# First tiles of a fused attention and mixture-of-experts kernel: no table for roots, decay loaded first, three clamps on VectorE, queries scaled ahead of a clamp, and unread turns of the unit matrix on TensorE

## The reference

```python
f = 1.0 / (1.0 + np.exp(-f_logit))                       # attention: B=4, H=8, S=768, D=48
for t in range(S):
    state = f[:, :, t, :, None] * state + np.einsum('bhd,bhe->bhde', k[:, :, t], v[:, :, t])
    y[:, :, t] = np.einsum('bhd,bhde->bhe', q[:, :, t], state)

xn = x / (np.linalg.norm(x, axis=-1, keepdims=True) + 1e-06)          # experts: E=8, rows of 384
en = expert_emb / (np.linalg.norm(expert_emb, axis=-1, keepdims=True) + 1e-06)
logits = xn @ en.T / tau
...
```

## Time and profile before

| what | value |
|---|---|
| median of 3 runs | 761.31 us (760.79 to 761.64) |
| the profiled execution, its own time | 764.95 us |
| its span, first to last instruction | 763.2 us |
| PE busy in the span | 724.4 us (95%) |
| DVE, ACT, POOL busy | 322.9, 281.6, 212.5 us |
| granted TensorE clock, mean of the span | 0.985 |
| attention stage | to about 154 us |

### The profile page before, as it was taken

The page is one execution under the profiler, slowest core; times in us unless marked ns, Lnnn a source line. Parts: engine busy times, 40 slices in busy tenths (PEclk is TensorE's granted clock), DMA queues, the critical chain, the costliest instruction groups (busy, mean ns, idle before and its releaser), DMA issues.

```text
span 763.2 us, 13668 instructions
## 1 busy us (share of the span) xinstructions
PE 724.4 (95%) x4832; PEld 646.6 (85%) x4832; DVE 322.9 (42%) x528; ACT 281.6 (37%) x520; POOL 212.5 (28%) x246
## 2 busy tenths in 40 slices
PE   4999999999479999999999989999999999999995
PEld 3999999856279999999999988898988988889885
DVE  5667777557135564564554651211211212112110
ACT  6666666423034354453453542302213022121220
POOL 7656756317700000000000002305224042141341
PEclk9999999999779999999999999999999999999998
DMA  8677885264824453552553451001000000000001
GB/s 252 183 230 212 267 231 136 75 187 152 283 54 125 124 166 96 152 165 82 159 153 100 132 146 55 1 1 41 1 17 24 0 31 10 4 38 0 21 21 41
DMA packets 78542, 79.51 MB, mean 104 GB/s; under 512 B 20688, under 2 KB 66776, under 8 KB 78512
## 3 DMA queue, kind: packets, MB, share of 16 engines
q1 hardware_dynamic: 75184, 68.88, 30.6%
q0 software_dynamic: 3328, 10.25, 3.7%
HBM read 64.09 MB, written 15.02 MB: 104 GB/s over the span
## 4 chain that ended last, share of the span: by engine, by line
PE 68%; issue 15%; POOL 11%; another core or an unknown queue 3%; ACT 1%; DVE 0%; POOLq 0%; DVEq 0%
PE bank L760 9%; PE bank L762 9%; PE bank L761 9%; POOL p_lo L583 7%; PE b_a L760 6%; PE b_a L761 6%; PE b_a L762 6%; PE b_a L620 4%; PE bank L629 3%; PE bank L660 3%; POOL out L588 3%; PE b_a L730 3%; PE bank L669 3%; PE bank L649 3%
## 5 line engine op out<-in xcount | busy, mean ns | idle before, releaser
L583 POOL TENSOR_TENSOR p_lo<-prod,p_hi 128x512 fp32r<-128x512 f32 x48 | 61.5, 1286 | 441.5 <-ACT p_hi L1003 441.5
L1000 ACT COPY a_sb<-b_a 128x512 f32<-128x512 f32 x48 | 28.3, 589 | 222.9 <-PE bank L762 222.9
L1335 DVE TENSOR_TENSOR prod<-bank,a_sb 128x512 f32<-128x512 f32 x48 | 33.2, 692 | 163.9 <-ACT a_sb L1000 163.9
L760 PE MATMUL b_a<-x_hi,w_hi 128*128 128x432 f32 x192 | 69.7, 363 | 15.3 <-DVE w_lo L1230 15.3
L965 ACT ACTIVATE h_hi<-b_a 128x432 fp32r<-128x432 f32 x64 | 34.1, 532 | 120.4 <-PE b_a L762 120.4
L1299 DVE SCALAR_TENSOR_TENSOR h_lo<-b_a,h_hi 128x432 fp32r<-128x432 f32 x64 | 38.9, 607 | 89.6 <-ACT h_hi L965 89.6
L1230 DVE TENSOR_TENSOR w_lo<-w_raw,w_hi 128x768 fp32r<-128x768 f32 x72 | 67.8, 957 | 6.6
L760 PE MATMUL bank<-h_hi,w_hi 128*128 128x432 f32 x192 | 70.1, 365 | 0.0
L761 PE MATMUL b_a<-x_lo,w_hi 128*128 128x432 f32 x192 | 69.5, 362 | 0.0
L762 PE MATMUL b_a<-x_hi,w_lo 128*128 128x432 f32 x192 | 69.4, 361 | 0.0
L762 PE MATMUL bank<-h_hi,w_lo 128*128 128x432 f32 x192 | 68.7, 358 | 0.0
(11 more groups left out here) (199 smaller groups left out, 1433.2 us busy)
## 6 DMA issues: line engine op xcount, KB each, us to landing
w_raw<-sets SPq DMA_DIRECT2D x80, 192.0 KB
w_raw<-sets SPq DMA_DIRECT2D x40, 384.0 KB
ring_all<-qkvf SPq DMA_DIRECT2D x24, 384.0 KB, 4.1
xs<-x_sorted SPq DMA_DIRECT2D x9, 772.0 KB, 6.0
ring_f<-qkvf SPq DMA_DIRECT2D x24, 192.0 KB, 4.0
ring_all<-qkvf SPq DMA_DIRECT2D x24, 192.0 KB, 3.2
x_recurrence<-x_all SPq DMA_DIRECT2D x24, 192.0 KB, 3.6
w_sb<-w_t SPq DMA_DIRECT2D x8, 512.0 KB, 4.9
```

What stands on the lines that cost most here:

```text
L583: pool.tensor_tensor(p_lo[:, f, :], prod[:, f % 2, :], p_hi[:, f, :].bitcast(F32), ALU.subtract).then_inc(pl_done, 1)
L760: pe.matmul(acc, a_hi, b_hi, start=first, stop=False, skip_group_check=skip)
L1000: act.copy(a_sb[:, f % 2, :], b_a[f % 2][:]).then_inc(as_done, 1)
L1335: dve.tensor_tensor(prod[:, f % 2, :], b_b[f % 2][:], a_sb[:, f % 2, :], ALU.mult).then_inc(pr_done, 1)
```

## The change

- The embedding is loaded fourth, not first. It lands in `x_tile`, with its squares in `rt`. The root is no longer ACT's Sqrt, so that one table load of ACT is gone: ACT takes Ln and Exp of half of it in step -1 (`guess_norm`), and DVE improves the guess in step 0 with one step of Newton's method and divides (`scale_emb`, seven instructions, five of them linked by a semaphore each). PE turns the embedding behind `turn_qk` of tile 1, not of tile 0.
- SP's order is decay of tile 0, queries and keys of tile 0, decay of tile 1, embedding, decay of tile 2. The load of `tau` and the four blocks of zeros stand behind the stages of tiles 4 to 7. The reciprocal of `tau` is taken on DVE behind all steps.
- DVE clamps tiles 0, 1 and 2, the first two right after its first memset. Tile 1's `low_logs` moves into step -2, behind `bound` of tile 0. POOL clamps from tile 3 on, so that `scale_q` of tile 0 is its first instruction behind the constants.
- ACT copies `qT` of tile 0 ahead of `exps` of tile 1.
- PE transposes the unit matrix into `b_x`, which nobody reads: 16 times at the start, 10 times between `cumulate` of tiles 0 and 1, and 8 times ahead of `turn_qk` of tile 0.

```diff
@@ -287,8 +287,6 @@
...
-        sp.dma_start(emb_sb, emb).then_inc(emb_in, 16)
...
@@ -337,10 +335,10 @@
...
         load_f(0, 0)
+        load_qk(0, 0)
         load_f(1, 1)
-        load_qk(0, 0)
+        sp.dma_start(emb_sb, emb).then_inc(emb_in, 16)
         load_f(2, 2)
-        sp.dma_start(tau_sb[:], tau).then_inc(small_in, 16)
         load_qk(1, 1)
         load_v(0, 0)
...
         load_v(RING - 1, RING - 1)
-        sp.wait_ge(pads_done, 3)
-        for i in range(SUB):
-            sp.dma_start(xs_dram[NTOK + i * P:NTOK + (i + 1) * P, :], zero_rows[:]).then_inc(zero_out, 16)
...
@@ -375,6 +370,10 @@
...
         four(1)
+        sp.dma_start(tau_sb[:], tau).then_inc(small_in, 16)
+        sp.wait_ge(pads_done, 3)
+        for i in range(SUB):
+            sp.dma_start(xs_dram[NTOK + i * P:NTOK + (i + 1) * P, :], zero_rows[:]).then_inc(zero_out, 16)
         with sp.Fori(2, NT // RING - 1) as m:
...
@@ -485,7 +484,7 @@
...
-            need(pool, lg_done, i if isinstance(i, int) and i == 2 else i - 1)
+            need(pool, lg_done, i if isinstance(i, int) and i == 3 else i - 1)
...
@@ -510,11 +509,11 @@
...
         def step(s, r):
-            if (i := tile_of(s, 3, 2)) is not None:
+            if (i := tile_of(s, 3, 3)) is not None:
                 before_clamp(i, r + 3)
             if (i := tile_of(s, -2)) is not None:
                 decay(i, r + 2)
-            if (i := tile_of(s, 3, 2)) is not None:
+            if (i := tile_of(s, 3, 3)) is not None:
                 clamp(i, r + 3)
             if (i := tile_of(s, 1)) is not None:
                 scale_q(i, r + 1)
@@ -604,6 +603,11 @@
...
+        def warm(n):
+
+            for _ in range(n):
+                pe.transpose(b_x[:, 0:P], ident[:], ident[:])
+
...
         def turn_emb():
 
-            pe.wait_ge(emb_step, 4)
+            pe.wait_ge(emb_scaled, 1)
...
         def step(s, r):
+            if isinstance(s, int) and s < 0:
+                warm({-3: 16, -2: 0, -1: 10}[s])
             if (i := tile_of(s, 0)) is not None:
                 scores(i, r)
             if (i := tile_of(s, 2)) is not None:
@@ -703,8 +709,9 @@
             if (i := tile_of(s, 1)) is not None:
                 if isinstance(i, int) and i == 0:
                     pe.wait_ge(pads_done, 1)
+                    warm(8)
                 turn_qk(i, r + 1)
-                if isinstance(i, int) and i == 0:
+                if isinstance(i, int) and i == 1:
                     turn_emb()
...
@@ -860,9 +867,6 @@
...
-        act.wait_ge(emb_step, 1)
-        act.activation(emb_n[:, 1:2], emb_n[:, 0:1], ACT.Sqrt).then_inc(emb_step, 1)
...
@@ -892,6 +896,13 @@
...
+        def guess_norm():
+
+            act.wait_ge(emb_step, 1)
+            act.activation(emb_n[:, 1:2], emb_n[:, 0:1], ACT.Ln).then_inc(emb_step, 1)
+            act.wait_ge(emb_step, 2)
+            act.activation(emb_n[:, 2:3], emb_n[:, 1:2], ACT.Exp, scale=0.5).then_inc(emb_step, 1)
...
                 copy_yT(i)
             if (i := tile_of(s, 3, 2)) is not None:
                 logs(i, r + 3)
+            if isinstance(s, int) and s == -1:
+                copy_qT(0, 0)
             if (i := tile_of(s, 2)) is not None:
                 exps(i, r + 2)
-            if (i := tile_of(s, 1)) is not None:
+            if isinstance(s, int) and s == -1:
+                guess_norm()
+            if (i := tile_of(s, 1, 1)) is not None:
                 copy_qT(i, r + 1)
...
@@ -1025,9 +1040,6 @@
...
-        dve.wait_ge(emb_in, 16)
-        dve.tensor_tensor_reduce(out=emb_sq, in0=emb_sb, in1=emb_sb, scale=1.0, scalar=0.0,
-                                 op0=ALU.mult, op1=ALU.add, accum_out=emb_n[:, 0:1]).then_inc(emb_step, 1)
...
@@ -1083,11 +1095,15 @@
...
-            if (i := tile_of(s, 3, 2)) is not None:
+            if (i := tile_of(s, 3, 1)) is not None:
                 low_logs(i, r + 3)
+            if isinstance(s, int) and s == -3:
+                first_clamp(2)
+            if isinstance(s, int) and s == 0:
+                scale_emb()
             if (i := tile_of(s, 1)) is not None:
                 copy_kT(i, r + 1)
-                if isinstance(i, int) and i == 0:
+                if isinstance(i, int) and i == 1:
                     take_emb()
...
         def first_clamp(i):
 
             dve.wait_ge(f_landed[i], 16)
-            dve.tensor_scalar_max(fc[:, i, :], ring_f[:, i, :], FLOOR).then_inc(clamp_done, 1)
+            need(dve, lg_done, i - 1)
+            dve.tensor_scalar_max(fc[:, i % 2, :], ring_f[:, i, :], FLOOR).then_inc(clamp_done, 1)
...
+        def scale_emb():
+
+            dve.wait_ge(emb_step, 3)
+            link(dve.reciprocal(emb_n[:, 3:4], emb_n[:, 2:3]))
+            link(dve.tensor_tensor(emb_n[:, 4:5], emb_n[:, 3:4], emb_n[:, 0:1], ALU.mult))
+            link(dve.tensor_tensor(emb_n[:, 5:6], emb_n[:, 4:5], emb_n[:, 2:3], ALU.add))
+            link(dve.tensor_scalar(emb_n[:, 6:7], emb_n[:, 5:6], 0.5, EPS_NORM, ALU.mult, ALU.add))
+            link(dve.reciprocal(emb_n[:, 7:8], emb_n[:, 6:7]))
+            dve.tensor_scalar(emb_pad[:, :, 0:D], emb_sb.rearrange("p (h d) -> p h d", h=H), emb_n[:, 7:8], None, ALU.mult)
+            dve.tensor_scalar(emb_sq, emb_sb, emb_n[:, 7:8], None, ALU.mult).then_inc(emb_scaled, 1)
+
         dve.memset(b_y[:], 0.0).then_inc(blank_done, 1)
+        first_clamp(0)
+        first_clamp(1)
         dve.memset(yT[:], 0.0).then_inc(blank_done, 1)
         dve.wait_ge(masks_done, 3)
         dve.tensor_copy(upto_r[:], upto[:])
-        first_clamp(0)
-        first_clamp(1)
         dve.tensor_copy(pick[:, :, 0:2 * D].rearrange("p j (g d) -> p j g d", g=2),
                         ident[:].rearrange("p (g d) -> p g d", g=2)[:, :, 0:D].unsqueeze(1).to_broadcast([P, NP, 2, D]))
-        dve.wait_ge(emb_step, 2)
-        link(dve.tensor_scalar_add(emb_n[:, 2:3], emb_n[:, 1:2], EPS_NORM))
-        dve.reciprocal(emb_n[:, 3:4], emb_n[:, 2:3]).then_inc(emb_step, 1)
         low_logs(0, 0)
-        dve.wait_ge(emb_step, 3)
-        dve.wait_ge(blank_done, 2)
-        dve.tensor_scalar(emb_pad[:, :, 0:D], emb_sb.rearrange("p (h d) -> p h d", h=H), emb_n[:, 3:4], None, ALU.mult)
-        dve.tensor_scalar(emb_sq, emb_sb, emb_n[:, 3:4], None, ALU.mult).then_inc(emb_step, 1)
-        low_logs(1, 1)
+        dve.wait_ge(emb_in, 16)
+        dve.tensor_tensor_reduce(out=emb_sq, in0=emb_sb, in1=emb_sb, scale=1.0, scalar=TINY,
+                                 op0=ALU.mult, op1=ALU.add, accum_out=emb_n[:, 0:1]).then_inc(emb_step, 1)
+        dve.wait_ge(pads_done, 2)
+        steps(dve, step)
+
+        dve.wait_ge(const_done, 1)
         dve.wait_ge(small_in, 16)
         link(dve.reciprocal(rtau[:], tau_sb[:]))
-        dve.wait_ge(pads_done, 2)
-        steps(dve, step)
-
-        dve.wait_ge(const_done, 1)
```

More of the change, by code:

```diff
@@ L56 @@
 EPS_SUM = 1e-9
+TINY = 1e-30
 RING = 4
@@ L161, in build @@
     en_t = early("en_t", [P, KD, E])
-    emb_sb = am[0:E, 0].rearrange("p j t -> p (j t)")[:, 0:DM]
-    emb_sq = am[0:E, 1].rearrange("p j t -> p (j t)")[:, 0:DM]
     emb_pad = yT[0:E, :].rearrange("p (h d) -> p h d", h=H)
-    emb_n = early("emb_n", [E, 4])
+    emb_n = early("emb_n", [E, 8])
     tau_sb = early("tau_sb", [P, 1])
@@ L181, in build @@
     zero_rows = early("zero_rows", [P, ROW])
+    emb_sb, emb_sq = x_tile[0:E, :], rt[0:E, 0:DM]
     x_rows = x_all[:, 0:NT * ROW]
@@ L251, in build @@
     masks_done, pads_done = sem("masks_done"), sem("pads_done")
-    const_one, const_done, emb_step, emb_turned, en_done = (sem(n) for n in (
-        "const_one", "const_done", "emb_step", "emb_turned", "en_done"))
+    const_one, const_done, emb_step, emb_scaled, emb_turned, en_done = (sem(n) for n in (
+        "const_one", "const_done", "emb_step", "emb_scaled", "emb_turned", "en_done"))
     clamp_done, ef_done, lg_done, ll_done, cum_done, bound_done, ec_done, exp_done = (sem(n) for n in (
@@ L1111, in _ @@
         dve.tensor_copy(upto_r[:], upto[:])
-        first_clamp(0)
-        first_clamp(1)
         dve.tensor_copy(pick[:, :, 0:2 * D].rearrange("p j (g d) -> p j g d", g=2),
                         ident[:].rearrange("p (g d) -> p g d", g=2)[:, :, 0:D].unsqueeze(1).to_broadcast([P, NP, 2, D]))
-        dve.wait_ge(emb_step, 2)
-        link(dve.tensor_scalar_add(emb_n[:, 2:3], emb_n[:, 1:2], EPS_NORM))
-        dve.reciprocal(emb_n[:, 3:4], emb_n[:, 2:3]).then_inc(emb_step, 1)
         low_logs(0, 0)
-        dve.wait_ge(emb_step, 3)
-        dve.wait_ge(blank_done, 2)
-        dve.tensor_scalar(emb_pad[:, :, 0:D], emb_sb.rearrange("p (h d) -> p h d", h=H), emb_n[:, 3:4], None, ALU.mult)
-        dve.tensor_scalar(emb_sq, emb_sb, emb_n[:, 3:4], None, ALU.mult).then_inc(emb_step, 1)
-        low_logs(1, 1)
-        dve.wait_ge(small_in, 16)
-        link(dve.reciprocal(rtau[:], tau_sb[:]))
+        dve.wait_ge(emb_in, 16)
+        dve.tensor_tensor_reduce(out=emb_sq, in0=emb_sb, in1=emb_sb, scale=1.0, scalar=TINY,
```

(3 more changed lines are left out.)

## The result

The changed kernel takes 766.82 us (median of 4 executions, 766.17 to 768.52), the kernel before 761.35 in the same session (4, 760.79 to 761.64): a ratio of 1.0077, with an interval of 1.0061 to 1.0093. Forecast were 760.1 and a range to 763.9, so the time lies outside it, on the slow side. The profiled execution took 766.59 with a span of 764.8.

The account below looks back on a forecast made before the run. TensorE bounds the kernel, busy 724.4 of 763.2 us. Scores of tile 1 1.4 us earlier plus 0.2 for 1/tau gave -1.2 us: 760.1 against the median 761.31, 8-in-10 range 759.1 to 763.9.

Parts of the forecast that it names:

- step 6: Embedding's new place: TensorE stands 2.65 us ahead of its turn; scores of tile 1 at 20.75, 1.4 us earlier.
- the premise that behind the scores of tile 1 nothing changes: Behind the start of tile 1's scores, engines have the work of before at TensorE's pace: 5.73 us per tile.
- Steps 1 to 3: Program start: third load at 5.8, sums at 7.6, `ec` at 9.3, queries at 9.45 in place of 10.56.
- step 2: VectorE to the first sums: GpSimd's constants, ending at 9.42, just cover the late clamp; loads later than 5.8 cost fully.
- The clock in the pause: Rival: clock rises early, falls in the pause ahead of the embedding's turn; products cost 1.0 more, 761.1; chance 0.10.
- Step 4: The 34 unread turns: first 16 free; the other 18 take 0.11 us each at high clock, 4.4 us at low.
- The rival built on that rule: Clock comes late or not from transposes: +2.8 to +3.8 us, 764.1 to 765.1; chance 0.15.
- Step 5: Tile 0 at high clock: turns 10.85 to 11.7, scores at 12.55 in place of 14.51, 1.95 us won.
- Step 7: The rest: zeros and `tau` moved to the middle are covered by load lead; 1/tau on VectorE adds 0.17 us.

Follow-up runs that it names:

- Experiment 4: Changed kernel with the decay of tile 1 loaded second, ahead of queries and keys of tile 0: ratio 1.0068 against the kernel before.
- experiment 6: Changed kernel with 24 more unread turns in TensorE's pause, right ahead of the embedding's turn: ratio 1.0106 against the kernel before.
- experiments 9: Changed kernel with the 10 and 8 turns taken out and 18 put into the pause ahead of the embedding's turn: ratio 1.0041 against the kernel before.
- 11: The kernel of numbers 10 with only the first 16 turns, without the 10 and the 8: ratio 1.0012 against the kernel before.
- number 7: Changed kernel with the embedding prepared one step earlier and decay of tile 1 loaded second: 758.83 us, ratio 0.9964 against the kernel before.
- experiment 12: Kernel before with the same 34 turns (16, 10, 8) and nothing else of the change: ratio 0.9976 against the kernel before.
- numbers 10: The kernel of number 7 with 1/tau taken on VectorE at the end of an earlier step: ratio 0.9964 against the kernel before.

## Why the prediction was wrong, point by point

**The step that failed is step 6 with what it left out of the clock,** and with it the premise that behind the scores of tile 1 nothing changes. The place and kind of the loss were right (a pause ahead of the embedding's turn, products and the copy of `kT` queued behind it), and so was the early clock. Against 20.75 for the scores of tile 1 the chain has 23.91, 3.16 more, and it splits into three:

- Steps 1 to 3, 0.67 (scores of tile 0 at 13.22, not 12.55). The third load was clamped at 6.29, not 5.8, inside its bounds. From there to the start of `lg_lo` it took 1.36 us, not 1.1, most of the difference in the copy of `pick` (0.46 on the path, counted at 0.27). `ec` ended at 10.0 for 9.3, and GpSimd's constants, the cover I named, were over at 8.75 for 9.42: it waited 1.35 us. Once the cover was gone each late tenth was on the path, as step 2 had said. Experiment 4 shows the price: up to 1.5 us at the sums. The landing itself isn't fixed: with this order of loads the clamp began between 4.97 and 6.29 in seven executions.
- Step 6's sum of operations, 0.9. From the scores of tile 0 to the embedding's turn it took 6.12 us, not 5.2. The mask began 0.5 late, behind VectorE's product for the keys of tile 1; the small operation beside GpSimd's product was 0.75 longer than the 0.15 of its neighbours; the two scalings took 0.75 where I had 1.02.
- The clock in the pause, 1.64. I gave it a chance of 0.10 and a price of 1.0; experiment 6 measured 1.64. The embedding's own turns were 0.60 (0.65 forecast). All three executions with a pause of 3.5 us show the fall; with this pause filled or gone, none has it there.

**Step 4** was right. The 16 turns raised the clock: sums of 0.44 us behind them, in eight of the ten executions with these turns. The Trainium skill ("TensorE: Matmul & The Clock Gate", Part 4: PE-mode transpose) says that the full clock does not engage for transposes; the measurement differs and decides. The rival built on that rule got 0.15 and foresaw a slower kernel, but by another way than the one that happened. Right, too, was that 10 and 8 turns cost little; that without them the clock is low again, or stays low, for tile 0 I had not seen (experiments 9 and 11).

**Step 5** had the turns (0.89), the 0.87 to the scores and the early rise. **Step 7** was right: from the scores of tile 1 to `least_e` it is 132.67 us against 132.50, so 1/tau cost its 0.2 and the zeros in the middle nothing. Wrong was the premise ahead of the steps, that behind tile 1 "the engines have the work of before": the loss at tile 1 is 2.5 us against the repeated kernel before, and the span's is 5.8. Apart from 1/tau it is two falls of the clock, at 157 and at 457. They can be read off as two levels. From the first dense matmul to the end it takes 307.5 to 307.7 us in seven executions, and 309.2 to 309.3 in six (309.2 in the changed kernel: 764.8 - 455.59); experiment 6 stands apart (310.1). Likewise it takes 1.6 to 1.7 us more in five of fourteen to a point 12 us behind `least_e`. This is the view of the windows with the fall and without it, in number 7 and in the repeat of before:

```profile
449.00:452.00 3.00, 3.00 (x9) 2.32 (x8) 0.00 (x0) 0.00 (x0) 0.00 (x0) 0.50 1.05 335
```

```profile
456.00:460.00 4.00, 4.00 (x19) 3.30 (x19) 0.69 (x1) 0.56 (x2) 0.00 (x0) 1.00 0.16 59
```

The sum against the repeat of before: 2.5 at tile 1, 0.2 for 1/tau, 1.5 from `least_e` to the dense groups (with the fall at 157) and 1.6 behind (with that at 457) make 5.8, the difference of the spans. Only the first two are shown to be the change's. The fast kernel of experiment 7 has the fall at 449 as well, the kernel before with turns (experiment 12) has both, and the two executions of the changed kernel differ in it; so whether the change makes these later falls more frequent, or this execution drew both, stays open. In the repeat of the changed kernel the loss at tile 1 was 4.3 and one later fall 1.7. Of the 6.7 us by which the forecast missed, then, step 6 and its neighbours hold 3.2, and most of the rest lies in these later falls, for which the sum had no term.

**The baseline.** I took -1.2 off a profiled execution that held a stand of 17 us on ScalarE, 3.5 us of it on the path. The difference was carried over, so the stand itself did no harm. But that execution also began 0.7 us later than its repeat (22.07 and 21.37 at tile 1), so half of the forecast gain of 1.4 was measured against a late start, and the one trace could not show that the clock's falls are drawn anew, and the earlier trace rows were read behind that stand.

## What to carry to other kernels

Filling work that raises TensorE's clock is worth only what the next pause leaves of it: look for the first place where TensorE waits, and move what it waits for (here seven small operations of VectorE, 4.8 us at tile 1) before adding any filler. When a pause is estimated, price its upper end with the work behind it at the low clock. And take two profiled executions before working with differences of 1 us, since the clock's falls behind equal pauses came in some and not in others, at 1.5 to 1.7 us each.

## What was not expected of the hardware

- Transposes of the unit matrix alone raised the granted clock: after 16 in 3.68 us, sums took 0.44 us, not the 0.66 to 0.69 without them. It was not certain: in one kernel two executions differed by the second sums (0.44 and 0.69), and in numbers 10 and 11 the first sums still took 0.69, where number 7, the same to that point, has 0.44.
- Pauses of 2.3 to 2.4 us ahead of the dense groups were followed by a low clock in six of thirteen executions, and two pauses of 0.7 to 1.1 us at the end of the attention in five of fourteen, at 1.5 to 1.7 us a time. At the dense groups the changed kernel's own two executions differ, with the same pause of 2.42; at the end of the attention both executions of the changed kernel have the fall and both of before have not.
- VectorE's operation on 8x1 took 0.90 to 0.92 us, not 0.15, in each of the six executions in which GpSimd's product of 128x384 had begun 0.1 us ahead of it, and 0.15 in the five where it had not.
- VectorE's cast of 128x128, begun at 4.93 beside GpSimd's memset of 128x1536 (4.57 to 5.95), took 1.10 us in three executions and 1.46 in a fourth; begun at 7.12, behind that memset, it took 0.16.
